# Second phase of an attention and two-layer kernel: block products by Strassen's scheme on pairs of token chunks

## The reference, cut to what matters

```python
# attention over 8 batches, 8 heads, 576 tokens, head size 64 -> x (8, 576, 512)
# first layer:  xk, xr = mixes of x and the token before
#               x2 = sigmoid(xr @ w_r) * (relu(xk @ w_k)**2 @ w_v)
def _moe2_ref(x, U, V, w_ch1, w_ch2):           # second layer, x is x2
    xt = x.transpose(0, 2, 1)
    h = xt @ U @ V                              # U 576x32, V 32x576
    u = x + h.transpose(0, 2, 1)
    ch = np.maximum(u @ w_ch1, 0.0) @ w_ch2     # 512 -> 2048 -> 512
    return (u + ch).astype(np.float32)
```

## Time and profile before

| | us |
|---|---|
| median of three runs | 1485.67 (1483.29 to 1488.79) |
| profiled execution | 1490.72, its span 1488.8 |
| PE busy | 1408.9 (95%), granted clock 0.991 |
| DVE busy | 571.1 (38%) |
| ACT busy | 425.6 (29%) |
| POOL busy | 41.7 (3%) |
| DMA | 76.09 MB, 51 GB/s over the span |

### The profile page before, as it was taken

How to read it: one execution, slowest core, us unless ns; L and a number is a source line. 1 busy time by engine, 2 the same in 40 slices (tenths; PEclk the granted TensorE clock), 3 DMA queues, 4 the chain that set the end, 5 groups by cost and what they waited for, 6 DMA issues and landing times.

```text
span 1488.8 us, 18181 instructions
## 1 busy us (share of the span) xinstructions
PE 1408.9 (95%) x7728; PEld 1173.2 (79%) x7728; DVE 571.1 (38%) x939; ACT 425.6 (29%) x734; POOL 41.7 (3%) x46
## 2 busy tenths in 40 slices
PE   2279999999999999999999999999999999999999
PEld 1168787788878888878888888888888888888887
DVE  2666667767666645444221211212111121211211
ACT  1445465464445444433111111111111110111110
POOL 2700000000000000000000000000000000000000
PEclk9989999999999999999999999999999999999999
DMA  7743243323332000233010010101001010010000
GB/s 141 182 84 68 66 87 77 93 41 84 64 83 47 13 28 22 84 126 121 29 64 0 31 34 0 64 1 61 3 1 64 0 64 1 6 52 0 29 1 29
DMA packets 194561, 76.09 MB, mean 51 GB/s; under 512 B 163056, under 2 KB 175376, under 8 KB 194480
## 3 DMA queue, kind: packets, MB, share of 16 engines
q1 hardware_dynamic: 186512, 67.76, 18.0%
q0 software_dynamic: 1632, 5.40, 1.2%
q10 hardware_dynamic: 6336, 1.77, 0.5%
HBM read 54.45 MB, written 20.45 MB: 50 GB/s over the span
## 4 chain that ended last, share of the span: by engine, by line
PE 86%; DVE 6%; SPq 4%; ACT 2%; issue 1%; DMA 1%; DVEq 0%; ACTq 0%
PE bank L1104 26%; PE bank L1074 26%; PE bank L644 12%; PE bank L658 10%; PE bank L623 5%; SPq L863 3%; DVE mixed L596 2%; PE bank L727 1%; PE bank L794 1%; SPq L877 1%; PE bank L443 1%; ACT mixed L583 1%; PE bank L798 1%; PE bank L399 1%; PE bank L1090 1%
## 5 line engine op out<-in xcount | busy, mean ns | idle before, releaser
L1252 DVE SCALAR_TENSOR_TENSOR hid_lo<-bank,hid_hi 128x512 fp32r<-128x512 f32 x144 | 99.6, 691 | 499.8 <-ACT hid_hi L1187 499.8
L1187 ACT ACTIVATE hid_hi<-bank 128x512 fp32r<-128x512 f32 x144 | 86.1, 598 | 600.1 <-PE bank L1104 600.1
L1104 PE MATMUL bank<-uT_hi,w_hi 128*128 128x512 f32 x576 | 224.9, 390 | 0.0
L1104 PE MATMUL bank<-uT_hi,w_lo 128*128 128x512 f32 x576 | 224.4, 390 | 0.0
L1104 PE MATMUL bank<-uT_lo,w_hi 128*128 128x512 f32 x576 | 224.4, 390 | 0.0
L1074 PE MATMUL bank<-w_hi,hid_lo 128*128 128x512 f32 x576 | 224.2, 389 | 0.0
L1074 PE MATMUL bank<-w_hi,hid_hi 128*128 128x512 f32 x576 | 224.1, 389 | 0.0
L1074 PE MATMUL bank<-w_lo,hid_hi 128*128 128x512 f32 x576 | 224.1, 389 | 0.0
L644 PE MATMUL bank<-xk_hi,wk_hi 128*128 128x384 f32 x384 | 132.6, 345 | 8.4 <-DVE xk_lo L615 8.4
L644 PE MATMUL bank<-xk_lo,wk_hi 128*128 128x384 f32 x384 | 130.1, 339 | 0.0
L644 PE MATMUL bank<-xk_hi,wk_lo 128*128 128x384 f32 x384 | 130.1, 339 | 0.0
(11 more groups left out here) (122 smaller groups left out, 1636.5 us busy)
## 6 DMA issues: line engine op xcount, KB each, us to landing
x_scratch<-x SPq DMA_DIRECT2D x36, 256.0 KB, 2.0
x_b<-x_scratch SPq DMA_DIRECT2D x9, 1024.0 KB, 6.1
out_dram<-x_b SPq DMA_DIRECT2D x36, 256.0 KB, 2.0
kq_parts<-in_k SPq DMA_DIRECT2D x120, 72.0 KB, 2.5
x_b<-in_moe_w_ch SPq DMA_DIRECT2D x16, 512.0 KB, 4.1
kq_parts<-in_q SPq DMA_DIRECT2D x112, 72.0 KB, 2.2
v_rows<-in_v SPq DMA_DIRECT2D x56, 128.0 KB
g<-g_scratch SPq DMA_DIRECT2D x16, 128.0 KB, 5.0
```

What stands on the lines that cost most here:

```text
L1104: last = nc.tensor.matmul(bank, w1s[a][:, ct, f * P:(f + 1) * P], uT[C % 2][b][:, ct, :], start=(ct == 0 and a == 0 and b == 0), stop=(ct ...
L1187: nc.scalar.activation(hid[0][:, f % RH, :], h_bank[(NFB * C + f) % 3], ACT.Relu).then_inc(h_hi, 1)
L1252: nc.vector.scalar_tensor_tensor(hid[1][:, f % RH, :], h_bank[(NFB * C + f) % 3], 0.0, hid[0][:, f % RH, :].bitcast(F32), ALU.max, ALU.sub ...
```

## The change

Phase A is the same but for its last group. Phase B becomes five pairs of chunks: three pairs of 2 x 512 tokens, two of 2 x 384.

For each pair, a product of 2 x 2 blocks (two halves of the contraction, two halves of the outputs, two chunks) is done with seven block products instead of eight, in Winograd's form: besides the blocks themselves there are four combinations (T1 to T4) of weight blocks, four of input blocks, and sums of the products. This is done for both layers. Hidden units are cut in two groups (g); in a group there are 4 units of 7 products in stage 1, and 7 products of 4 entries in stage 2. Every product or entry is 6 matmuls with one weight entry of 256 KB.

- **Weights.** 32 pieces are loaded, combined by four POOL additions, split by ACT and DVE and stored to DRAM tensors w1_parts and w2_parts. 24 pieces stand in the slots of phase A's last group, 8 in the first pair. In phase B every product streams its entry from there through a ring of 10 buffers; the load of entry e + 10 is issued behind product e.
- **Stage 1.** Products T2, T3 and T4 accumulate onto a bank which ACT or DVE has just read; ACT and DVE form the four hidden blocks (ea, ez, eb, c11, c22, c12, c21, relu), DVE four combinations (t), and then ACT and DVE split the seven.
- **Stage 2.** The same for the second layer; 16 DVE sums per group go into an accumulator in SBUF, which starts as a copy of u. L1090 and L1266 are gone.
- **u.** 40 groups instead of 36. POOL forms combinations of u, ACT and DVE split seven parts of two tiles, in the second half of the pair before.
- **Output.** The accumulator holds the output transposed in 32 x 32 blocks after a DVE transpose; SP stores each of 8 tiles per pair with four DMAs of 128-byte rows.

The diff, cut to its core:

```diff
-CB, TPB = 512, 4
-NB = B * S // CB
+PAIRS_B = ((0, 512), (1024, 512), (2048, 512), (3072, 384), (3840, 384))
+NB = len(PAIRS_B)
+NG, NU = 2, 4
+NPROD = 7
+PIECES = 2 * 2 * NG * NU
+LATE = PIECES // 4
+SLOTS_P = 3
+RW, RH = 10, 3
...
+def piece_items():
+    plan = {}
+    for i in range(PIECES - LATE):
+        at = 3 * i // 2
+        plan.setdefault(at, []).append(("ws_load", i))
+        plan.setdefault(at + 2, []).append(("ws_split", i))
+        plan.setdefault(at + 3, []).append(("ws_store", i))
+    return plan
+LATE_SPOTS = [(0, i, pos) for i in range(1, NU) for pos in (1, 3, 5)] + [(1, 0, 2), (1, 0, 4)]
+def late_pieces(spot):
+    at = LATE_SPOTS.index(spot)
...
+    for kind, after in (("ws_split", 2), ("ws_store", 3), ("ws_load", 0)):
...
+def pair_plan(p, left, turns):
+    for g in range(NG):
+        for i in range(NU):
+            for pos in range(NPROD):
+                items.append(("m1", g, i, pos))
...
+                if pos in (2, 3) and turns:
+                    items += turns.pop(0)
...
+                if g == 1 and p < NB - 1 and pos in (1, 4):
+                    n = 2 * i + pos // 4
+                    items.append(("u", p + 1, n))
+                    if n == 3:
+                        items.append(("x_load", p + 1, 1))
...
+        for e in range(NPROD * NU):
+            pos, i = divmod(e, NU)
+            items.append(("m2", g, pos, i))
...
+            if e + RH < NPROD * NU:
+                items.append(("split", g, e + RH))
+            if ready:
+                items += ready.pop(0)
...
+            if g == NG - 1 and p < NB - 1 and e % 2 == 1:
+                items.append(("us", p + 1, e // 2))
...
+    def pool_u(pool, p):
...
+            nc.gpsimd.tensor_tensor(u_t[:, 1, ct, 0:w], a[:, ct, 1, 0:w], a[:, ct, 0, 0:w],
+                                    ALU.subtract).then_inc(u_sum, 1)
...
+    def pe_m1(pe, p, g, i, pos):
+        pe.wait_ge(ring_in[e % RW], 16 * (e // RW + 1))
...
+        elif pos == T2:
+            pe.wait_ge(p1_ok, no + 1)
+        elif pos == T3:
+            pe.wait_ge(b_ok, no + 1)
+        elif pos == R22:
+            pe.wait_ge(c11_ok, no + 1)
+        elif pos == T4:
+            pe.wait_ge(c22_ok, no + 1)
+        to = role(st, side, BANK_OF[pos])[:, 0:w]
+        for ct in range(2):
+            for a, b in ((0, 0), (0, 1), (1, 0)):
+                last = nc.tensor.matmul(to, wring[:, e % RW, ct, a, :], uc[:, pos, b, ct, 0:w],
...
+    def dve_turn_out(dve, p, k):
...
+            dve.wait_ge(out_done[no % 2], 64 * (no // 2))
...
+    def pool_piece(pool, n):
+        pool.wait_ge(piece_in[slot], ...)
+        nc.gpsimd.tensor_tensor(r[:, 2, :], r[:, 0, :], r[:, 7, :], ALU.add).then_inc(piece_sum, 1)
+        nc.gpsimd.tensor_tensor(r[:, 5, :], r[:, 1, :], r[:, 0, :], ALU.subtract).then_inc(piece_sum, 1)
+        pool.wait_ge(piece_sum, 4 * n + 1)
+        nc.gpsimd.tensor_tensor(r[:, 3, :], r[:, 2, :], r[:, 1, :], ALU.subtract).then_inc(piece_sum, 1)
+        pool.wait_ge(piece_sum, 4 * n + 3)
+        nc.gpsimd.tensor_tensor(r[:, 6, :], r[:, 4, :], r[:, 3, :], ALU.subtract).then_inc(piece_sum, 1)
+    def act_piece(act, n):
+        act.wait_ge(piece_sum, 4 * n + 4)
+        ge(act, piece_stored[slot], 16 * turn)
+        nc.scalar.activation(piece_out[slot][:, :, 0, :], piece_raw[slot][:, 1:NPROD + 1, :], ACT.Copy)...
+        def load_piece(n):
+            ge(sp, piece_lo, n - SLOTS_P + 1 if n < early else n - 1 if n > early + 1 else 0)
...
+        def store_piece(n):
+            sp.wait_ge(piece_lo, n + 1)
...
+        def load_ring(e):
+            ge(sp, prod_ps, e - RW + 1)
...
+            sp.dma_start(wring[:, e % RW, :, :, :]..., part...).then_inc(ring_in[e % RW], 16)
+        def load_x2(p, half):
+            if p > 0:
+                sp.wait_ge(u_ps, 2 * CT * p + CT * half)
...
+            elif item[0] == "out":
...
+                for quad in range(4):
+                    to = out.rearrange("b s d -> (b s) d")[lo:lo + w, nt * P + 32 * quad:nt * P + 32 * quad + 32]
+                    sp.dma_start(to.rearrange("(m t) d -> t m d", t=32),
+                                 turned[no % 2][32 * quad:32 * quad + 32, 0:w].rearrange("t (m d) -> t m d", d=32)
```

More of the change, by code:

```diff
@@ L208, in ge, with b_plan @@
+def b_plan():
+    items = []
+    left, turns = [], []
+    for p in range(NB):
+        own, left, turns = pair_plan(p, left, turns)
+        items += [(p, item) for item in own]
+    return items
 def ge(eng, sem, value):
@@ L824, in dve_bw, with tokens, batches_of, unit @@
-    def dve_bw(dve, i):
-        src, dst, a = b_chunks[i]
-        dve.wait_ge(bw_hi, i + 1)
-        nc.vector.tensor_tensor(dst[1], parts(stage_b[i % RB], a), dst[0].bitcast(F32),
-                                ALU.subtract).then_inc(bw_lo, 1)
+    def tokens(p, half):
+        start, w = PAIRS_B[p]
+        return start + half * w, w
+    def batches_of(p, half):
+        lo, w = tokens(p, half)
+        return range(lo // S, (lo + w - 1) // S + 1)
+    def unit(p, g, i):
+        return NU * (NG * p + g) + i
@@ new lines, in split_no, with sum_no, pe_u @@
+    def split_no(p, g, e):
+        return NPROD * NU * (NG * p + g) + e
+    def sum_no(p, g, k):
+        return NSUM * (NG * p + g) + k
+    def pe_u(pe, p, n):
+        half, ct = divmod(n, CT)
+        lo, w = tokens(p, half)
+        no = 2 * CT * p + n
+        ge(pe, u_raw, no - 1)
+        if ct == 0:
+            pe.wait_ge(x2_in[half], 16 * (p + 1))
+            pe.wait_ge(g_in, 32 * (batches_of(p, half)[-1] + 1))
+        tiles = x2_t[1 if (p, half) == (0, 1) else 0]
+        for t in range(w // P):
+            nc.tensor.matmul(u_bank[n % 2][:, t * P:(t + 1) * P], tiles[:, t, ct * P:(ct + 1) * P], ident[:, :],
+                             start=(t == 0), stop=False, is_transpose=True)
+        for b in batches_of(p, half):
+            a, z = max(lo, S * b) - lo, min(lo + w, S * (b + 1)) - lo
+            col = PAD + lo + a - S * b
+            last = nc.tensor.matmul(u_bank[n % 2][:, a:z], g4[b % 2][:, ct * P:(ct + 1) * P],
+                                    v4[:, col:col + z - a], start=False, stop=(b == batches_of(p, half)[-1]))
+        last.then_inc(u_ps, 1)
@@ new lines, in pe_m2 @@
+    def pe_m2(pe, p, g, pos, i):
+        st, w = 2 * (NG * p + g) + 1, PAIRS_B[p][1]
+        e, no = entry(p, g, pos, i, 1), split_no(p, g, NU * pos + i)
+        final, base = unit(p, g, NU - 1) + 1, sum_no(p, g, 0)
+        pe.wait_ge(ring_in[e % RW], 16 * (e // RW + 1))
+        pe.wait_ge(hid_lo, no + 1)
+        if i == 0:
+            if pos == R11:
+                pe.wait_ge(p5_ok, final)
+            elif pos == T1:
+                pe.wait_ge(c12_ok, final)
+            elif pos == R21:
+                pe.wait_ge(c21_ok, final)
+            else:
+                before = {T2: R11, T3: T2, R22: R21, T4: T3}[pos]
+                pe.wait_ge(sum_ok, base + SUM_AT[READY[before][-1]] + 1)
+        for j in range(2):
+            for a, b in ((0, 0), (0, 1), (1, 0)):
+                last = nc.tensor.matmul(role(st, j, BANK_OF[pos])[:, 0:w], wring[:, e % RW, j, a, :],
+                                        hid[:, no % RH, b, 0:w],
+                                        start=(pos in FRESH and i == 0 and a == 0 and b == 0),
+                                        stop=(i == NU - 1 and a == 1), skip_group_check=(pos in CHAIN))
+        last.then_inc(prod_ps, 1)
@@ L844, in everything @@
                 do_a(item, PAIRS - 1, c)
-        for C in range(NB):
-            for item in hidden_plan(C):
-                do_b(item, C)
+        for p, item in b_plan():
+            do_b(item, p)
     block = ctx.enter_context(nc.Block())
@@ new lines, in load_x2 @@
+        def load_x2(p, half):
+            lo, w = tokens(p, half)
+            if p > 0:
+                sp.wait_ge(u_ps, 2 * CT * p + CT * half)
+            before = batches_of(p, 0) if half else batches_of(p - 1, 1) if p > 0 else ()
+            for b in batches_of(p, half):
+                if b not in before:
+                    sp.wait_ge(g_out, 16 * (b + 2))
+                    ge(sp, g_in, 32 * b)
+                    load_g(b, b % 2)
+            for s in x2_out:
+                sp.wait_ge(s, 16 * (NCH + 1 if p > 0 else 4))
+            rows = x2_dram[lo:lo + w, :].rearrange("(t p) d -> p t d", p=P)
+            sp.dma_start(x2_t[1 if (p, half) == (0, 1) else 0][:, 0:w // P, :], rows).then_inc(x2_in[half], 16)
@@ L1065, in do_a @@
                 pe_g(pe, g + item[3], item[1], item[2])
[L1066 to L1067 removed]
+            elif item[0] == "u":
+                if item[2] == 0:
                     pe.wait_ge(v_lo, 1)
                     pe.wait_ge(v_pad, 2)
[L1070 to L1076 removed]
```

650 lines of the change are left out of this document (414 added, 236 removed), and 3 rows, old and new, of the table where.

## The result

The changed kernel takes 1510.97 us (median of 4 runs, 1509.66 to 1514.17), the kernel before 1486.02 in the same comparison: ratio 1.0163, 95% interval 1.0143 to 1.0184. It is 1.6% slower; the forecast was 1458, 1.9% faster. The time lies inside the stated range of 1403 to 1512, by one microsecond, but on the other side of no change.

What follows compares the result with a forecast made beforehand. The prediction took TensorE's matmuls to bound the second phase (work for 816.9 of 817.2 us). Terms -103 + 37 + 10 + 0 + 10 + 8 + 6 + 4 = -28 took 1490.7 to 1462.7, less 5: 1458; range 1403 to 1512.

Steps and rivals of the forecast that it cites:

- Part 1: Second phase: fewer matmuls through seven products, and L1090's matmuls gone; u groups taken as 0 extra: -103 us.
- Part 2: Last group of phase A: 24 weight pieces set the pace at 5.45 us each, u starts later: +37 us.
- Part 3: First pair: the other 8 weight pieces, with two buffers and beside the ring: +10 us, bounds +3 and +22.
- Part 4: Second phase: ring loads of weight entries are covered by DMA rate and ten slots: 0 us.
- Part 5: u of the next pair: second x2 tile late by 2.3 to 2.5 us in four pairs: +10, bounds 0 and +20.
- Part 6: Output stores in 128-byte rows, first quarter of the next pair: hidden at 512, not fully at 384: +8, bounds 0 and 30.
- Part 7: Second half of a pair: VectorE barely hidden, POOL additions beside it; +6 us over four pairs, bounds 0 and 16.
- Part 8: Seam before the first product +1, tail of sums, turn and short-row stores +3: together +4 us.
- ring rival: Second phase: ring entries come one at a time at 172 GB/s, total about 1590, mild form 1495 to 1520; chance 0.18.
- exclusion rival: POOL and DVE exclude each other everywhere, piece loop 12.7 us: +6, 1491 or no change; chance 0.15.

Runs made afterwards that it cites:

- e8: Changed kernel with the edits of e1, e2, e3, e4 and e5 together, correct or not: 1431.1 us, ratio 0.963.
- e1: Changed kernel with, in phase A, the load of piece n issued ahead of the store of piece n-2: 1488.2 us, ratio 1.0013.
- e2: Changed kernel without the eight late pieces; the ring reads group 0's w2 parts for both groups (output wrong): 1487.5 us, ratio 1.000.
- e6: Changed kernel with late pieces at every fourth product from the ninth on, next pair's x2 load behind them: 1502.7 us, ratio 1.0105.
- e9: Changed kernel with the edits of e1, e3 and e6, and each late piece's store at the spot of its split: 1461.3 us, ratio 0.9816.
- e3: Changed kernel with the next pair's first four u groups in unit 0 of group 1, second x2 tile requested earlier: 1498.5 us, ratio 1.0079.
- e5: Changed kernel with output DMAs writing the same bytes in rows of 384 or 512 elements, not 32 (wrong order): 1495.9 us, ratio 1.0077.
- e10: e9 with a ring of 8 weight slots in place of 10 and four row buffers in place of two: 1468.7 us, ratio 0.9845.
- e4: Changed kernel with POOL's additions for u of pairs 2 to 4 on 32 columns (output partly wrong): 1502.0 us, ratio 1.010.
- e12: e9 with GpSimd's queue issuing two of each tile's four output DMAs in the last pair: 1463.3 us, ratio 0.9844.

## Why the prediction was wrong

The forecast sum was -28, the profiled executions show +20.1. The difference of 48 comes from the covered costs, not from the gain or the largest price. What failed is the overlap assumed in parts 3, 5, 6, 7 and 8: each was priced as mostly hidden, and each came out above its value. Part by part:

- **Part 1 (-103) was right.** Pair 2's group 0 runs at 38.1 and 38.6 against 38.1, the first multiplication of the last pair's group 1 at 29.2 against 29.1. With five costs off (e8) the phase is 88.9 us shorter than before, window to window. One slip had little weight: the second phase before holds 32 u groups and not 36 (the first four run before 668.7), so its sum is 813.6 and leaves 3.6 us of 817.2 unplaced, not 0.9.
- **Part 2 (+37) was right** in size: 5.24 us a piece for 5.45, last split at 657.8 for 660, u at 674.2 for 676, +35.1. ScalarE waits for POOL's sums in 22 places, as forecast. e1 shows the issue order to be 16.7 of the 35.1; for the rest the loop as written is argued and not shown. The price of 40.8 until the first product adds the four u groups that now stand ahead of it (8 for 4, 2.6 us, which part 1 had taken as 0) and 2.0 us at the seam, for which part 8 had 1; 1.1 us is not placed.
- **Part 3 (+10) failed first**: 23.5 by e2, just over its bound of 22. The step that failed is "the store is issued before the piece that the load waits for, so the loop is shorter". The order does take the store out of the load's loop, but by putting it a spot later, behind the load and ring entries (734.85 and 737.88 above). With two output buffers the piece after next can't be split before it has landed, so ScalarE waited 17.7 us for stores with TensorE's evacuations behind it. e6 moved the wait, e9 removed most of it by moving each store four products forward; it did so on top of e6 and not at the pieces' first places.
- **Part 4 (0) was right with nothing to spare**: 10 slots show 5.9 us of ring waits in e9, 8 slots 18.0 and +7.1 us. The waits of the changed kernel, 5.4 us, are all in the narrow pairs, as forecast.
- **Part 5 (+10)** is 12.5 by e3; excess of the four stages beyond their u groups (8 x 0.66 in each pair) is 35.2 - 21.1 = 14.1. Mechanism right, size a little low: the group could start 6.0 us after SyncE took up the request, where four products are 5.4, and the g loads ahead of it took 2.04 to issue; two of the four gaps were followed by half clock.
- **Part 6 (+8)** is the largest miss in kind: 15.1 by e5, and group 0 of pairs 1 to 4 exceeds its products by 24.1. I added the DMA's bytes up over a quarter pair and let nine ring entries absorb the overrun. What happened is local: four issues of these stores stretch to 1.35 us on average (0.59 over all 160), SyncE then issues the ring's loads late, and the turns wait for one of two buffers on VectorE ahead of the evacuations. Which of the two counts is not separated: in e10 two more buffers moved the wait to a ring of 8 and gave nothing. The 8 us of the 24.1 that are left with wide rows stay open. The Trainium skill ("DMA: Bandwidth & Descriptors", Specifications) says that below 512 B the DMA does a read-modify-write. That wider rows give back 15.1 us agrees with it, though no run here separates this from the number of packets.
- **Part 7 (+6)** is 14.2 by the stages (4.1, 4.1, 2.2, 3.8); e4 gives back 9.0 with three of the four pairs' POOL work shrunk, 6.8 of it in these stages. Five POOL operations fall in that time in pair 0, where the part has four. The bound of 16 held; the value was taken too near to zero for an engine at 34.2 of 38.1 us, in which every stretched operation shows. The Trainium skill ("SBUF — State Buffer", Who interferes with whom) has it that a VectorE instruction with two SBUF inputs contends with a GpSimd instruction that reads SBUF. The rows at 870.72 and 872.11 agree: 1.47 and 1.77 us for 0.68.
- **Part 8 (+4)**: seam 2.0, tail 7.7. The tail's 32 issues, 0.51 us apart, run for 16.9 us from 1490.27 on, a count that I had made for the middle of the kernel and not for its end. But e12 halved SyncE's count and the tail stayed, so this count alone does not explain it.

Together: late pieces 24 for 10, x2 tile 14 for 10, second halves 14 for 6, group 0 of the later pairs 24 for 8, the last pair's end 1: 77 for 34 in the second phase, +43; the tail +5. (The start's 2.8 us over the forecast and 3 us more gain in the phase, since four of the u groups stand ahead of it, cancel.) These 48 turn -28 into +20. Of the 77, TensorE stands for 47 and loses some 13 to the half clock, for which the sum had no term, only the upper bound of part 5. The other 17 don't show as idle: the modelled ends of matmuls (0.39 us for one that starts every 0.2267) cover short delays. Of the rivals none came true as written. The mild form of the ring rival named the right time (1495 to 1520) with the wrong cause: TensorE waited only 5.4 us for the ring. That the time lies in the stated range at all is luck, at its far end and on the wrong side of no change. The exclusion rival was right in part 7 but not in the piece loop. The common error is that each hidden cost was priced by its own work against the room left, near its lower bound, while all of them share a few in-order queues (SyncE, VectorE, ScalarE) and use up the same room: all five of the smaller ones came out above the value.
